# Fused attention and two MLPs: quarter tiles in the first stage, scores of all groups ahead, fourth group of the first tile turned sooner

## The chip, the cores and the metric

One core of a Trainium2 chip runs the whole program. The metric is the time of one execution on the device, in microseconds (us).

## The reference

Attention on q, k and v of shape 8 x 8 x 576 x 64 (batch, heads, tokens, head width), within chunks of 64 tokens, and then two MLPs on the 4608 x 512 result:

```
scores = (q_c @ k_c.T) / sqrt(64)          # per head and chunk: 64 x 64
attn   = exp(scores - max); attn /= sum(attn) + 1e-9
x      = attn @ v_c                        # heads side by side: 4608 x 512
x      = relu(x @ w_in)**2 @ w_out         # 512 -> 2048 -> 512
h      = x @ w2_in
g      = where(h >= 1, h, where(h <= -1, 0, (h + 1)**2 / 4))
out    = g @ w2_out
```

## The kernel before

**Tiles and groups.** The 4608 tokens are nine tiles (TILES) of 512. A tile has four groups (GROUPS) of 128 tokens, a group has two chunks. Every large product is made of three passes, since each operand is held as a high part (HI, rounded to fp32r) and a low part (LO, the rest): ScalarE writes the high part, VectorE (for weights GpSimd) subtracts it to get the low one. In an MLP the hidden width is 16 slices (FT) of 128. `up` (L392) makes one slice of the hidden layer in one of two PSUM banks (`h_ps`), ScalarE takes relu and square (L689, L693, L694), VectorE the low part (`hid_lo`, L917), and `down` (L430) adds the slice's part of the output into the four banks of `acc`. up of the next slice is issued ahead of down of the one before. Phase 0 is the first MLP (tiles 0 to 8), phase 1 the second.

**Attention inside the tiles.** While tile t goes through the first MLP, the attention of tile t + 1 is made in its gaps, a group in four slices: exponentials on ScalarE (L632), `normalise` on VectorE (L876), `turn_probs` (L888, eight 32-row transposes of the probabilities in two halves, part 0 and part 1), then `heads_and_scores` on TensorE: 16 matmuls of 64x64 for the head outputs (L507; each f32 matmul shows as two instructions) and 16 for the scores of the next group (L520). VectorE's `turn` (L813) transposes q and k of the next groups, 16 transposes cut up by TURNS. In tile 0 the steps are laid out by STEPS_OF_FIRST_TILE, and its fourth group has parts 0 and 1 in one slice, f = 13. There VectorE runs in this order: normalise; hid_lo of slice 13; turn_probs part 0; nine transposes of q and k; hid_lo of slice 14; turn_probs part 1; four transposes; hid_lo of slice 15. TensorE's heads wait for the second half of turn_probs, and the scores behind them for the transposes of q and k and for hid_lo of slice 15.

**The first stage.** Before there is an MLP to hide it, the attention of groups 0 to 3 (tile 0) and the scores of group 4 are made with TensorE as transposer. After the matmuls of `keep_up` and a warming loop (L443, L572) the program order of TensorE is written out by hand: `turn(g)` (L462) transposes q and k of a group into acc banks 0 and 1; `score(g)` (L473) makes the scores into one bank, `s_ps`, as 8 matmuls of 128 x 64 x 128: k is stored zero-padded, so that q of two heads meets the even head's k and the odd head's k side by side (`qk_t` with three planes: q, even k, odd k). ScalarE copies q (L641) and the odd heads' half of k (L645), VectorE the even half (`copy_k`, L822). VectorE takes the maximum (`take_max`, L834) and subtracts it (`shift`, L841), ScalarE exponentiates (L651), VectorE sums (L849) and inverts (L866, L868), GpSimd normalises groups 0 to 2 (L324) and VectorE group 3 (L876). TensorE turns the probabilities (`turn_probs`, L486), ScalarE copies the two 64-row halves onto the diagonal blocks of a zeroed tile (`copy_turned`, L661; the second half of group 3 is VectorE's, L967), and `head_out` (L534) multiplies with v, 8 matmuls of 128 x 64 x 128. The result goes into `x_t`: high part on ScalarE (L679), low part on VectorE (L780), which count up x_hi and x_lo.

The order of TensorE is: score(0), turn(1), score(1), turn(2), turn_probs(0), score(2), turn(3), turn_probs(1), head_out(0), score(3), head_out(1), turn_probs(2), turn(4), up_half(0, 0), turn_probs(3), head_out(2), head_out(3), up_half(1, 0), up_half(0, 1), score(4), up_half(1, 1). `up_half(f, part)` (L403) is half of up for slice f, on the tokens of groups 0 and 1 (part 0) or 2 and 3 (part 1), 12 matmuls. up_half(0, 0) waits for x_lo of groups 0 and 1 and for w_in slice 0; up_half(1, 0) for w_in slice 1. Then down of slice 0 begins, which waits for its hid_lo.

**Buffers.** Probabilities are in `probs` (even groups) and `probs_spare` (odd groups), the turned ones in the upper half of `v_and_probs` and in `raw`. q and k of group 2 arrive in two parts of `stage`, which is also where the weights land (w_in slices in planes 0 and 2, w_out in 1 and 3).

**Queues.** GpSimd issues the weight loads and does their low parts (L313, L318), in one written order with the normalisations; its first load waits for the second turning (`k_turned`). SP issues q, k and v. ScalarE casts the weights' high parts (L616, L622), in its own written order: weights_in(0) between the heads of groups 0 and 1, weights_in(1) right after copy_turned(2).

## Time and profile before

| | |
|---|---|
| Time, median of 3 runs | 1646.14 us (1645.05 to 1646.54) |
| The profiled execution | 1645.59 us, of which the span of the profile is 1643.8 us |
| TensorE busy | 1635.7 us, 9354 matmul instructions |
| VectorE, ScalarE, GpSimd busy | 870.5, 597.3, 130.5 us |
| Granted TensorE clock | 1.00 (full) in all slices of the span |

Times in the rows are microseconds from the span's start. A row of a timeline merges instructions of one kind that follow each other: start, length, engine, line, operation, output <- inputs, shapes and count; in square brackets the idle time of the engine before it and what ended it. PE is TensorE's matmuls and PEld its weight loads, DVE VectorE, ACT ScalarE, POOL GpSimd, SP SyncE. The busy share of an engine says little by itself here; what counts is which wait ends last at a given place.

### The profile page before, as it was taken

How to read it: one execution, taken by the hardware profiler on the slowest of the kernel's cores; microseconds unless marked ns; L12 is line 12 of the kernel's file. 1: busy time of each engine (PE TensorE's matmuls, PEld its weight loads, DVE VectorE, ACT ScalarE, POOL GpSimd, SP SyncE). 2: the span in 40 equal slices, each digit the busy share in tenths (PEclk: the TensorE clock that was granted, in tenths of full speed). 3: DMA queues.
4: the chain of work that ended last, by engine and by line, in shares of the span. 5: the costliest groups of instructions: out<-in, count | busy, mean ns of one | idle time of the engine just before them, and what ended most of it. 6: DMA issues, size and time to landing. Idle time of an engine off the chain costs nothing.

```text
span 1643.8 us, 24537 instructions
## 1 busy us (share of the span) xinstructions
PE 1635.7 (100%) x9354; PEld 1350.7 (82%) x9354; DVE 870.5 (53%) x1628; ACT 597.3 (36%) x1409; POOL 130.5 (8%) x138
## 2 busy tenths in 40 slices
PE   9999999999999999999999999999999999999999
PEld 8878888888888888888888888888888888888887
DVE  6777667666677666663124444443434344443433
ACT  5554444444444443444542222222222222222222
POOL 4740000000000000001660000000000000000000
PEclk9999999999999999999999999999999999999999
DMA  9532121112112121212321010101010101010000
GB/s 184 128 88 58 40 65 34 52 39 65 40 23 61 39 65 33 52 27 84 93 83 49 1 52 0 52 0 51 0 51 0 51 0 51 0 51 1 23 4 26
DMA packets 126654, 74.70 MB, mean 45 GB/s; under 512 B 115553, under 2 KB 115553, under 8 KB 124257
## 3 DMA queue, kind: packets, MB, share of 16 engines
q1 hardware_dynamic: 119328, 56.11, 12.9%
q0 software_dynamic: 5120, 16.78, 3.4%
q8 instruction: 63, 1.03, 0.3%
q10 hardware_dynamic: 2112, 0.52, 0.2%
q14 instruction: 31, 0.25, 0.1%
HBM read 54.53 MB, written 18.87 MB: 45 GB/s over the span
## 4 chain that ended last, share of the span: by engine, by line
PE 98%; DVE 1%; issue 0%; ACT 0%; POOL 0%; POOLq 0%; DVEq 0%
PE _out_and_h_and_scores_ps L392 47%; PE acc L434 24%; PE acc L430 24%; PE _out_and_h_and_scores_ps L507 1%; PE _out_and_h_and_scores_ps L520 1%; DVE q_t_and_k_t_by_head L813 0%; PE _out_and_h_and_scores_ps L403 0%; PE _out_and_h_and_scores_ps L473 0%; DVE v_and_probs_diag L888 0%; PE _out_and_h_and_scores_ps L443 0%; PE acc L486 0%; PE acc L462 0%; PE _out_and_h_and_scores_ps L572 0%; PE _out_and_h_and_scores_ps L534 0%; DVE hidden_split L917 0%
## 5 line engine op out<-in xcount | busy, mean ns | idle before, releaser
L392 PE MATMUL _out_and_h_and_scores_ps<-x_t_split,w_in_split 128*128 128x512 f32 x3432 | 819.3, 389 | 0.1
L392 PEld LDWEIGHTS _out_and_h_and_scores_ps<-x_t_split,w_in_split 128*128 128x128 f32 x3432 | 644.0, 188 | 134.6 <-DVE x_t_split L787 0.9
L430 PE MATMUL acc<-hidden_split,w_out_split 128*128 128x512 f32 x1728 | 419.6, 392 | 1.0 <-DVE hidden_split L917 1.0
L434 PE MATMUL acc<-w_out_split,hidden_split 128*128 128x512 f32 x1728 | 414.7, 389 | 0.0
L434 PEld LDWEIGHTS acc<-w_out_split,hidden_split 128*128 128x128 f32 x1728 | 324.3, 188 | 67.3
L430 PEld LDWEIGHTS acc<-hidden_split,w_out_split 128*128 128x128 f32 x1728 | 321.7, 188 | 69.5 <-issue 1.5
L909 DVE SCALAR_TENSOR_TENSOR hidden_raw<-hidden_raw 128x512 f32<-128x512 f32 x144 | 99.7, 692 | 348.9 <-ACT hidden_raw L698 348.9
L813 DVE STREAM_TRANSPOSE q_t_and_k_t_by_head<-qk_in 32x256 f32<-32x256 f32 x496 | 216.0, 435 | 7.4
L698 ACT ACTIVATE hidden_raw<-_out_and_h_and_scores_ps 128x512 f32<-128x512 f32 x144 | 86.1, 598 | 364.9 <-PE _out_and_h_and_scores_ps L392 364.9
L917 DVE TENSOR_TENSOR hidden_split<-_out_and_h_and_scores_ps,hidden_split 128x512 fp32r<-128x512 f32 x144 | 99.6, 692 | 219.9 <-ACT _out_and_h_and_scores_ps L694 219.3
L689 ACT ACTIVATE _out_and_h_and_scores_ps<-_out_and_h_and_scores_ps 128x512 f32<-128x512 f32 x144 | 83.8, 582 | 359.2 <-PE _out_and_h_and_scores_ps L392 357.2
L702 ACT CAST hidden_split<-hidden_raw 128x512 fp32r<-128x512 f32 x144 | 89.3, 620 | 214.3 <-DVE hidden_raw L912 212.2
L917 DVE TENSOR_TENSOR hidden_split<-hidden_raw,hidden_split 128x512 fp32r<-128x512 f32 x144 | 99.8, 693 | 99.5 <-ACT hidden_split L702 99.5
L888 DVE STREAM_TRANSPOSE v_and_probs_diag<-probs 32x256 f32<-32x256 f32 x256 | 111.4, 435 | 3.6
L912 DVE TENSOR_TENSOR hidden_raw<-_out_and_h_and_scores_ps,hidden_raw 128x512 f32<-128x512 f32 x144 | 99.5, 691 | 4.9
L693 ACT ACTIVATE hidden_split<-_out_and_h_and_scores_ps 128x512 fp32r<-128x512 f32 x144 | 86.4, 600 | 4.8
L694 ACT ACTIVATE _out_and_h_and_scores_ps<-_out_and_h_and_scores_ps 128x512 f32<-128x512 f32 x144 | 85.5, 594 | 0.0
L632 ACT ACTIVATE probs<-_out_and_h_and_scores_ps,exp_bias 128x64 f32<-128x64 f32 x248 | 74.1, 325 | 29.1 <-DVE exp_bias L860 29.1
L300 POOL DMA_DIRECT2D qk_in<-in_moe_w_in_dram x16 | 12.3, 768 | 632.4 <-DVE q_t_and_k_t_by_head L813 628.2
L632 ACT ACTIVATION_READ_ACCUMULATOR probs<-_out_and_h_and_scores_ps,exp_bias 128x1 f32 x248 | 53.9, 217 | 0.0
L855 DVE TENSOR_REDUCE score_max<-_out_and_h_and_scores_ps 128x8 f32<-128x512 f32 x31 | 21.4, 692 | 41.3 <-PE _out_and_h_and_scores_ps L520 41.3
L674 ACT CAST x_t_split<-_out_and_h_and_scores_ps 128x512 fp32r<-128x512 f32 x32 | 18.8, 586 | 51.6 <-PE _out_and_h_and_scores_ps L507 51.6
(80 smaller groups left out, 493.2 us busy)
## 6 DMA issues: line engine op xcount, KB each, us to landing
v_and_probs_diag<-in_v_dram SPq DMA_DIRECT2D x72, 128.0 KB, 3.0
mlp_out_t<-stage SPq DMA_DIRECT2D x9, 1024.0 KB, 4.3
v_and_probs_diag<-mlp_out_t SPq DMA_DIRECT2D x9, 1024.0 KB, 6.9
qk_in<-in_q_dram SPq DMA_DIRECT2D x68, 128.0 KB, 3.1
qk_in<-in_k_dram SPq DMA_DIRECT2D x68, 128.0 KB, 3.1
out_dram<-stage SPq DMA_DIRECT2D x8, 1024.0 KB, 5.2
stage<-in_moe_w_in_dram POOLq DMA_DIRECT2D x16, 256.0 KB, 3.3
stage<-in_moe_w_out_dram POOLq DMA_DIRECT2D x16, 256.0 KB, 3.0
```

The costliest lines, as they stand in the source:

```text
L392: last = nc.tensor.matmul(h_ps[:, bank, :], w_in[:, kt, w, cols], x_t[:, par, x, kt, :], start=(kt == 0 and w == HI and x == HI), stop=(kt ...
L430: last = nc.tensor.matmul(acc[:, j, :], w_out[:, f, w, cols], hid[:, half, x, :], start=first, stop=end)
L434: last = nc.tensor.matmul(acc[:, j, :], hid[:, half, w, cols], w_out[:, f, x, :], start=first, stop=end)
L632: last = nc.scalar.activation(probs_of(n)[:, pair, keys], scores[:, head % 2, pair, :], ACT.Exp, scale=SCALE, bias=bias[:, par, head:head ...
L693: nc.scalar.activation(hid[:, half, HI, :], squares, ACT.Square).then_inc(hid_hi, 1)
L698: nc.scalar.activation(raw[:, half, :], h_ps[:, half, :], ACT.Relu, bias=0.5, scale=0.5).then_inc(relu_done, 1)
L702: nc.scalar.copy(hid[:, half, HI, :], squares).then_inc(hid_hi, 1)
L813: last = nc.vector.transpose(dst, src)
L888: last = nc.vector.transpose(probs_diag[at:at + BLK, :, tok * BLK:(tok + 1) * BLK], heads[tok * BLK:(tok + 1) * BLK, :, wid * BLK:(wid + 1 ...
L909: nc.vector.scalar_tensor_tensor(out=a, in0=a, scalar=1.0, in1=a, op0=ALU.min, op1=ALU.mult).then_inc(squared, 1)
L912: nc.vector.tensor_tensor(a, h_ps[:, half, :], a, ALU.max).then_inc(raw_ready, 1)
L917: nc.vector.tensor_tensor(hid[:, half, LO, :], squares, hid[:, half, HI, :].bitcast(F32), ALU.subtract).then_inc(hid_lo, 1)
```

## The change

It rewrites the first stage, and moves one step in tile 0.

- k is stored unpadded (`qk_t` has two planes), the turned probabilities too. Scores and heads of the first stage use the 64 x 64 quarter tiles which the later tiles use already (`scores`, `heads`), 16 matmuls each, into pairs of banks. Nothing has to be zeroed.
- Each group 0 to 3 has a buffer of its own for its probabilities (`probs`, two of `probs_spare`, plane 3 of `stage`); q and k of group 2 arrive in `raw`.
- TensorE's order is now: score(0), turn(1), score(1), turn(2), score(2), turn(3), score(3), turn_probs(0), head_out(0), turn_probs(1), head_out(1), turn_probs(2), up_half(0, 0), turn_probs(3), head_out(2), turn(4), head_out(3), up_half(1, 0), up_half(0, 1), score(4), up_half(1, 1). Head outputs of groups 0 and 1 share one pair of banks, those of groups 2 and 3 another, and scores of groups 0 to 3 one.
- ScalarE copies q and all of k from group 1 on; VectorE copies k of group 0 alone. The written orders of ScalarE, VectorE and GpSimd follow; load_in(0) waits for the third turning, load_out(1) for turn_probs(2).
- In tile 0, shift(4) comes ahead of hid_lo of slice 0. Where parts 0 and 1 fall in one slice (the fourth group, f = 13), turn_probs part 0 comes right behind normalise, ahead of hid_lo.

The core of the diff; left out are the renaming of PSUM banks (same banks for the later tiles), of semaphores, and the moves of functions without a change in what they issue.

```diff
-        v_and_probs = sb("v_and_probs_diag", [P, 4, H * D])
+        v_and_probs = sb("v_and_probs_t", [P, 4, H * D])
...
-        probs_diag = v_and_probs[:, 2:4, :].rearrange("p a (h n) -> p (a h) n", n=P)
-        qk_t = sb("q_t_and_k_t_by_head", [P, HP, 3, P])
+        qk_t = sb("q_t_and_k_t", [P, HP, 2, P])
         probs = sb("probs", [P, HP, P])
-        probs_spare = sb("probs_spare", [P, HP, P])
+        probs_spare = sb("probs_spare", [P, 2, HP, P])
...
         def probs_of(n):
-            return probs_spare[:] if spare(n) else probs[:]
-
-        def probs_diag_of(n):
-            return raw[:].rearrange("p a (h n) -> p (a h) n", n=P) if spare(n) else probs_diag
+            if isinstance(n, int) and 1 <= n < GROUPS:
+                return stage[:, 3, :].rearrange("p (hp n) -> p hp n", n=P) if n == 2 else probs_spare[:, n // 2, :, :]
+            return probs[:]
+
+        def probs_t_of(n):
+            place = 3 if isinstance(n, int) and n < GROUPS and n % 2 == 1 else 2
+            return v_and_probs[:, place, :].rearrange("p (h n) -> p h n", n=CHUNK)
...
         def qk_of(g):
             if g == 2:
-                return stage[:, 1:4:2, :]
+                return raw[:]
             return qk_in[:, 0 if g in (0, 3) else 1, :, :]
...
+        def pair(first):
+            return banks[:, first:first + 2, 0:TILE // 2].rearrange("p a (hp n) -> p a hp n", n=CHUNK)
...
+        def early_scores(n):
+            return pair(2 if n == GROUPS else 6)
+
+        def early_heads_out(n):
+            return pair(4 if n < 2 else 3)
...
-            nc.gpsimd.memset(probs_diag_of(1), 0.0).then_inc(spare_zero, 1)
-            pool.wait_ge(k_turned, 2)
+            pool.wait_ge(k_turned, 3)
             load_in(0, 0, stage)
             normalise(0, 0)
+            load_in(1, 0, stage)
             normalise(1, 1)
-            load_in(1, 0, stage)
+            load_out(0, 0, stage)
             normalise(2, 0)
             weights_in(0, 0, stage)
-            pool.wait_ge(k_turned, 3)
-            load_out(0, 0, stage)
             load_in(2, 0, stage)
+            weights_in(1, 0, stage)
+            pool.wait_ge(p_turned, 3)
             load_out(1, 0, stage)
-            weights_in(1, 0, stage)
             load_in(3, 0, stage)
             weights_out(0, 0, stage)
             load_out(2, 0, stage)
...
+                if f == 1:
+                    pe.wait_ge(shifted, GROUPS)
...
+                    if not past(s, 1) and j == 2:
+                        pe.wait_ge(shifted, GROUPS + 1)
...
-                if g > 0:
-                    pe.wait_ge(q_copied, g)
-                    pe.wait_ge(k_copied, g)
-                for which, turned in ((0, q_turned), (1, k_turned)):
+                for which, turned, copied in ((0, q_turned, q_copied), (1, k_turned, k_copied)):
+                    if g > 0:
+                        pe.wait_ge(copied, g)
...
+            def scores(place):
+
+                for hp in range(HP):
+                    for r in range(2):
+                        head_rows = slice(r * D, (r + 1) * D)
+                        for c in range(2):
+                            rows = slice(c * CHUNK, (c + 1) * CHUNK)
+                            last = nc.tensor.matmul(place[rows, r, hp, :], qk_t[head_rows, hp, 0, rows],
+                                                    qk_t[head_rows, hp, 1, rows], start=True, stop=True)
+                last.then_inc(scored, 1)
...
+            def early_score(n):
                 pe.wait_ge(q_copied, n + 1)
                 pe.wait_ge(k_copied, n + 1)
+                if n == GROUPS:
+                    pe.wait_ge(p_copied, n)
+                    pe.wait_ge(x_lo, n)
+                elif n > 0:
+                    pe.wait_ge(shifted, n)
+                scores(early_scores(n))
...
+            def early_head_out(n):
+                pe.wait_ge(p_copied, n + 1)
                 if n > 0:
-                    pe.wait_ge(shifted, n)
-                for hp in range(HP):
-                    for c in range(2):
-                        rows = slice(c * CHUNK, (c + 1) * CHUNK)
-                        last = nc.tensor.matmul(s_ps[rows, hp, :], qk_t[:, hp, 0, rows], qk_t[:, hp, 1:3, rows],
-                                                start=True, stop=True)
-                last.then_inc(scored, 1)
+                    pe.wait_ge(x_lo, n)
+                heads(n, early_heads_out(n))
...
             keep_up(WARM[2])
-            for g in range(GROUPS):
-                score(g)
-                if g + 1 < GROUPS:
-                    turn(g + 1)
-                    if g == 0:
-                        keep_up(WARM[3])
-                    if g >= 1:
-                        turn_probs(g - 1)
-                    if g >= 2:
-                        head_out(g - 2, g % 2)
-            head_out(1, 1)
+            early_score(0)
+            turn(1)
+            keep_up(WARM[3])
+            early_score(1)
+            turn(2)
+            early_score(2)
+            turn(3)
+            early_score(3)
+            turn_probs(0)
+            early_head_out(0)
+            turn_probs(1)
+            early_head_out(1)
             turn_probs(2)
-            turn(GROUPS)
             up_half(0, 0)
             turn_probs(3)
-            head_out(2, 0)
-            head_out(3, 1)
+            early_head_out(2)
+            turn(GROUPS)
+            early_head_out(3)
             up_half(1, 0)
             up_half(0, 1)
-            score(GROUPS)
+            early_score(GROUPS)
...
-                nc.scalar.copy(qk_t[:, :, 0, :], acc[:, 0, :].rearrange("p (hp n) -> p hp n", hp=HP))
+                nc.scalar.copy(qk_t[:, :, 0, :], acc[:, 0, :].rearrange("p (hp n) -> p hp n", hp=HP)).then_inc(q_copied, 1)
+
+            def copy_k(g):
                 act.wait_ge(k_turned, g + 1)
-                if g == 0:
-                    act.wait_ge(k_zero, 1)
-                nc.scalar.copy(qk_t[D:2 * D, :, 2, :], acc[D:2 * D, 1, :].rearrange(
-                    "p (hp n) -> p hp n", hp=HP)).then_inc(q_copied, 1)
+                nc.scalar.copy(qk_t[:, :, 1, :], acc[:, 1, :].rearrange("p (hp n) -> p hp n", hp=HP)).then_inc(k_copied, 1)
...
-            def copy_turned(n, chunks=(0, 1)):
+            def copy_turned(n):
                 act.wait_ge(p_turned, n + 1)
                 if n >= 2:
                     act.wait_ge(headed, n - 1)
-                else:
-                    act.wait_ge(spare_zero if spare(n) else probs_diag_zero, 1)
-                for c in chunks:
-                    rows = slice(c * CHUNK, (c + 1) * CHUNK)
-                    last = nc.scalar.copy(probs_diag_of(n)[rows, :, rows], acc[rows, 2, :].rearrange("p (h n) -> p h n", n=CHUNK))
-                last.then_inc(p_copied, 1)
+                nc.scalar.copy(probs_t_of(n), acc[:, 2, :].rearrange("p (h n) -> p h n", n=CHUNK)).then_inc(p_copied, 1)
...
             copy_q(0)
-            for g in range(GROUPS):
-                if g + 1 < GROUPS:
-                    copy_q(g + 1)
-                if g == GROUPS - 1:
-                    x_in_hi(0, 0, 0)
-                    weights_in(0, 0, stage)
-                    x_in_hi(1, 0, 1)
-                exponentiate(g)
-                if g >= 1:
-                    copy_turned(g - 1)
+            copy_q(1)
+            copy_k(1)
+            exponentiate(0)
+            copy_q(2)
+            copy_k(2)
+            exponentiate(1)
+            copy_q(3)
+            copy_k(3)
+            exponentiate(2)
+            copy_turned(0)
+            heads_in_hi(0, 0, 0, early_heads_out(0))
+            exponentiate(3)
+            copy_turned(1)
+            weights_in(0, 0, stage)
+            heads_in_hi(1, 0, 1, early_heads_out(1))
+            copy_turned(2)
+            copy_turned(3)
+            heads_in_hi(2, 0, 2, early_heads_out(2))
             weights_in(1, 0, stage)
-            copy_turned(3, (0,))
-            x_in_hi(2, 0, 2)
-            x_in_hi(3, 0, 3)
+            heads_in_hi(3, 0, 3, early_heads_out(3))
+            copy_q(GROUPS)
+            copy_k(GROUPS)
...
             def shift(n):
                 dve.wait_ge(maxed, n + 1)
-                if n >= 2:
-                    dve.wait_ge(p_turned, n - 1)
-                nc.vector.tensor_tensor(probs_of(n).rearrange(by_head, n=CHUNK), s_ps.rearrange(by_head, n=CHUNK),
-                                        top[:].unsqueeze(2).to_broadcast([P, H, CHUNK]), ALU.subtract).then_inc(shifted, 1)
+                if n == GROUPS:
+                    dve.wait_ge(p_turned, 1)
+                nc.vector.tensor_tensor(
+                    probs_of(n).rearrange("p hp (r n) -> p r hp n", r=2), early_scores(n),
+                    top[:].rearrange("p (hp r) -> p r hp", r=2).unsqueeze(3).to_broadcast([P, 2, HP, CHUNK]),
+                    ALU.subtract).then_inc(shifted, 1)
...
                         normalise(n, g % 2)
+                        if 1 in parts:
+                            turn_probs(n, 0)
+                    if attends and begins:
+                        shift(n)
...
                     if attends and begins:
-                        shift(n)
                         turn(t, 1, 1, TURNS[0], TURNS[1])
...
                     for r in (1, 2):
-                        if attends and r in parts:
+                        if attends and r in parts and 0 not in parts:
                             turn_probs(n, r - 1)
...
-            nc.vector.memset(qk_t[:, :, 1:3, :], 0.0).then_inc(k_zero, 1)
-            nc.vector.memset(probs_diag, 0.0).then_inc(probs_diag_zero, 1)
-            dve.wait_ge(k_zero, 1)
-
-            copy_k(0)
+            dve.wait_ge(k_turned, 1)
+            nc.vector.tensor_copy(qk_t[:, :, 1, :], acc[:, 1, :].rearrange("p (hp n) -> p hp n", hp=HP)).then_inc(k_copied, 1)
             for g in range(GROUPS):
                 take_max(g)
                 shift(g)
-                if g + 1 < GROUPS:
-                    copy_k(g + 1)
-                    add_up(g, g % 2)
-                    invert(g, g % 2)
-            x_in_lo(0, 0, 0)
-            x_in_lo(1, 0, 1)
+                if g >= 1:
+                    add_up(g - 1, (g - 1) % 2)
+                    invert(g - 1, (g - 1) % 2)
+            heads_in_lo(0, 0, 0, early_heads_out(0))
             add_up(3, 1)
             normalise(3, 1)
-            dve.wait_ge(p_turned, 4)
-            dve.wait_ge(headed, 2)
-            nc.vector.tensor_copy(probs_diag_of(3)[CHUNK:P, :, CHUNK:P],
-                                  acc[CHUNK:P, 2, :].rearrange("p (h n) -> p h n", n=CHUNK)).then_inc(last_p_copied, 1)
-            copy_k(GROUPS)
-            x_in_lo(2, 0, 2)
-            x_in_lo(3, 0, 3)
-            copy_q_of_fifth()
+            heads_in_lo(1, 0, 1, early_heads_out(1))
+            heads_in_lo(2, 0, 2, early_heads_out(2))
+            heads_in_lo(3, 0, 3, early_heads_out(3))
```

## Rows read from the trace of the kernel before

**Rows 1.** Busy time of each engine in three stretches (length, busy, instructions; PEclk, DMA share, GB/s)

```profile
core 0: us, PE busy (x) PEld busy (x) DVE busy (x) ACT busy (x) POOL busy (x), PEclk, DMA share, GB/s
200.00:800.00 600.00, 600.00 (x4073) 493.09 (x4072) 390.23 (x843) 260.78 (x747) 18.81 (x21) 1.00 0.19 49
11.50:23.95 12.45, 11.28 (x205) 10.09 (x204) 10.47 (x22) 10.04 (x18) 6.85 (x8) 1.00 0.90 176
109.70:124.30 14.60, 12.90 (x115) 10.15 (x114) 13.27 (x31) 6.64 (x22) 3.71 (x3) 1.00 0.08 19
```

**Rows 2.** Timeline of TensorE in the first stage (start, length)

```profile
1.54 2.50 PE L443 MATMUL _out_and_h_and_scores_ps<-ident 128*128 128x128 f32 x10 [1.54 <-POOL ident L329]
...
8.95 1.09 PE L473 MATMUL _out_and_h_and_scores_ps<-q_t_and_k_t_by_head 128*64 128x128 f32 x16 [0.27 <-DVE q_t_and_k_t_by_head L822]
9.97 1.10 PE L462 MATMUL acc<-ident,qk_in 128*128 128x128 f32 x8
...
19.94 1.04 PE L473 MATMUL _out_and_h_and_scores_ps<-q_t_and_k_t_by_head 128*64 128x128 f32 x16
...
23.70 1.69 PE L403 MATMUL _out_and_h_and_scores_ps<-x_t_split,w_in_split 128*128 128x256 f32 x12
25.47 1.15 PE L486 MATMUL acc<-ident,probs_spare 128*64 128x64 f32 x32
...
28.48 3.17 PE L403 MATMUL _out_and_h_and_scores_ps<-x_t_split,w_in_split 128*128 128x256 f32 x24
...
34.33 3.00 PE L430 MATMUL acc<-hidden_split,w_out_split 128*128 128x512 f32 x12
```

**Rows 3.** Timeline of VectorE and TensorE around the fourth group of tile 0

```profile
105.79 0.69 DVE L876 TENSOR_TENSOR probs<-probs,prob_sum_inverse 128x512 f32<-128x512 f32 x1
...
109.07 0.69 DVE L917 TENSOR_TENSOR hidden_split<-_out_and_h_and_scores_ps,hidden_split 128x512 fp32r<-128x512 f32 x1 [2.59 <-ACT _out_and_h_and_scores_ps L694]
...
111.46 4.03 DVE L813 STREAM_TRANSPOSE q_t_and_k_t_by_head<-qk_in 32x256 f32<-32x256 f32 x9
...
115.50 0.69 DVE L917 TENSOR_TENSOR hidden_split<-_out_and_h_and_scores_ps,hidden_split 128x512 fp32r<-128x512 f32 x1
...
116.34 3.00 PE L430 MATMUL acc<-hidden_split,w_out_split 128*128 128x512 f32 x12 [0.95 <-DVE hidden_split L917]
...
119.88 0.69 DVE L917 TENSOR_TENSOR hidden_split<-_out_and_h_and_scores_ps,hidden_split 128x512 fp32r<-128x512 f32 x1
...
120.72 0.69 PE L520 MATMUL _out_and_h_and_scores_ps<-q_t_and_k_t_by_head 64*64 64x64 f32 x32 [0.75 <-DVE hidden_split L917]
```

**Rows 4.** Timeline of TensorE: quarter tiles inside tile 0

```profile
53.58 0.69 PE L507 MATMUL _out_and_h_and_scores_ps<-v_and_probs_diag 64*64 64x64 f32 x32
54.10 0.65 PE L520 MATMUL _out_and_h_and_scores_ps<-q_t_and_k_t_by_head 64*64 64x64 f32 x32
```

**Rows 5.** Timeline of ScalarE in the first stage

```profile
10.67 0.59 ACT L641 COPY q_t_and_k_t_by_head<-acc 128x512 f32<-128x512 f32 x1 [2.05 <-PE acc L462]
...
21.90 0.59 ACT L679 CAST x_t_split<-acc 128x512 fp32r<-128x512 f32 x1 [0.25 <-PE acc L534]
...
22.48 0.63 ACT L651 ACTIVATE probs_spare<-probs_spare 128x512 f32<-128x512 f32 x1
...
24.20 0.62 ACT L616 CAST w_in_split<-stage 128x512 fp32r<-128x512 f32 x1
...
31.69 0.58 ACT L689 ACTIVATE _out_and_h_and_scores_ps<-_out_and_h_and_scores_ps 128x512 f32<-128x512 f32 x1 [1.99 <-PE _out_and_h_and_scores_ps L403]
```

**Rows 6.** Timeline of VectorE in the first stage

```profile
10.81 0.69 DVE L841 TENSOR_TENSOR probs<-_out_and_h_and_scores_ps,score_max 128x512 f32<-128x512 f32 x1
...
22.96 0.68 DVE L780 TENSOR_TENSOR x_t_split<-acc,x_t_split 128x512 fp32r<-128x512 f32 x1
...
33.49 0.69 DVE L917 TENSOR_TENSOR hidden_split<-_out_and_h_and_scores_ps,hidden_split 128x512 fp32r<-128x512 f32 x1
```

**Rows 7.** Timeline of GpSimd: low part of one w_in slice

```profile
21.73 1.28 POOL L313 TENSOR_TENSOR w_in_split<-stage,w_in_split 128x512 fp32r<-128x512 f32 x1
```

**Rows 8.** Instructions of L300 (w_in loads) in the first 45 us: their landing times

```profile
DMA to landing us min/median/max: 3.2/4.5/6.3
```

124 lines of the change are left out of this document (38 added, 86 removed).

## The prediction, made before the change was run

> **What bounds the kernel now.** I read the stretches first, to see where TensorE has room. In the long middle it has none: it is busy 600.00 of 600.00 us, at the granted clock 1.00, which is the 2.4 GHz level [rows 1]. So nothing the change does on other engines can be seen there, and any microsecond lost or won before or between the dense blocks goes through to the end whole. The change touches two places. The first is the opening stage (attention of groups 0 to 3), which ends when the first down projection starts at 34.33 us [rows 2]; from 11.50 to 23.95 us TensorE is busy 11.28 of 12.45 us [rows 1], so the room there is about 1.2 us of idling plus whatever work is removed. The second is the fourth group in tile 0, where TensorE stands twice, 0.95 and 0.75 us, each time released by VectorE's hid_lo at L917 [rows 3]; the stretch around it is busy 12.90 of 14.60 us [rows 1]. Then I read the timeline of each engine for durations.
>
> **First stage, front half: the scores run ahead.** A padded score takes 1.09 us, and the turning behind it starts 1.02 later (8.95 and 9.97) [rows 2]. Quarter tiles, the form that L507 and L520 already have, take 0.69 and 0.65 us, the next starts 0.52 and 0.57 us after them [rows 4]. I take 0.57 for a score or a head_out. The opening up to score(0) at 8.95 is the same: the copy of k still sits on VectorE there, and the zeroing that is removed (DVE, POOL) was done before its operands arrived. Then, per group: the turning starts 0.57 after the score; ScalarE's copy of q starts 0.70 after the turning (9.97, 10.67) [rows 2, 5]; it now copies q and the whole of k one behind the other, 0.59 + 0.02 each (before, VectorE took half of k in parallel, but ScalarE's half cost it as much); 0.1 to TensorE. That is 0.57 + 0.70 + 1.20 + 0.10 = 2.57 per group. Scores of groups 1, 2, 3 start at 11.5, 14.05, 16.6 us; before, the last of them stood at 19.94 [rows 2]. VectorE's subtraction takes 0.69 [rows 6], and I give the max the same; they are done 2.1 us after a score starts, so they don't gate this cycle.
>
> **First stage, middle.** turn_probs(0) now stands behind score(3): 17.15 to 18.30 (1.15, as [rows 2] have it). From there TensorE has nothing to do in its written order but follow ScalarE's: copy_turned(0) to 18.93; head_out(0) 19.1 to 19.8; heads_in_hi(0), 0.59 [rows 5], to 20.4; then exponentiate(3), 0.63 [rows 5], which was ready at 18.7 but is queued behind it, to 21.04; copy_turned(1) to 21.65; head_out(1) 21.8 to 22.5; heads_in_hi(1) to 23.12; heads_in_lo(1), 0.68 [rows 6], to 23.85; up_half(0, 0) at 23.95. Before it started at 23.70 [rows 2]. So 3.3 us of lead in the scores are given back, and 0.25 us more. The cast of w_in(0), which waits for its transfer, is not in this way: load_in(0) is moved behind the third turning (to 13.2 us), its slowest landing is 6.3 us [rows 8], so it is there at about 19.6 to 20.5, and ScalarE asks for it at 21.67. Should the landing be later than that, each microsecond of it goes onto the end. SP's queue keeps its order; v and the fifth group are issued when they were, or earlier.
>
> **First stage, tail.** Before, TensorE was nearly dense from 25.47 to 34.33 us. Now: up_half(0, 0) to 25.5 (24 of these matmuls take 3.17, the last 0.07 beside what follows, so 12 take 1.55) [rows 2]; turn_probs(3) to 26.65; head_out(2); turn(4), which is moved to here and costs 1.1 (the eight matmuls at 9.97), to 28.3. head_out(3) has to wait, since groups 2 and 3 now share one place in PSUM: copy_turned(3) 26.7 to 27.3, heads_in_hi(2) to 27.97, heads_in_lo(2) to 28.7, so it starts at 28.8: **0.5 us idle**. ScalarE casts w_in(1) only behind heads_in_hi(2): 28.0 to 28.61 (0.62) [rows 5], GpSimd's part takes 1.28 [rows 7], so up_half(1, 0) starts at 30.0 instead of 29.4: **0.6 us idle**; it started at 28.48 before [rows 2]. Then up_half(0, 1) 31.6 to 33.15, and the relu at L689 follows at 33.2 (31.69 before) [rows 5]. Its hid_lo would be ready at 35.0, by the 1.80 us between 31.69 and 33.49 [rows 5, 6], but shift(4) is moved ahead of it on VectorE: score(4) at 33.15, max 33.88 to 34.57, subtraction to 35.28, hid_lo 35.3 to 36.0, down(0, 0) at 36.1. The first stage ends **1.8 us later** than at 34.33. The new wait at j = 2 of down(0, 0) and the one ahead of up_half(1) are long met. Moved later on POOL: load_out(1), to about 30.3, because weights_in(1) stands in front of it; with a landing of up to 6.3 us [rows 8] it is there at 36.6 to 37, just where ScalarE wants it (about 36.1), and down(0, 1) wants it at 41.8: I cost it at nothing, covered by 3 us.
>
> Bounds of this part: if the two idle spots of the tail and the shift are hidden after all, and the middle breaks even, +0.3; if each of some fourteen handovers costs 0.1 us more than I gave it, +3.2. I take 1.8, since all of its terms are durations of the same operations in this trace.
>
> **Fourth group of tile 0.** Before, VectorE ended its normalisation at 106.48 (105.79 + 0.69) and idled until hid_lo(13), then did four transposes of probabilities and nine of q and k at 0.45 each, and reached hid_lo(14) at 115.50, hid_lo(15) at 119.88 [rows 3]. The change puts the first four into that idle time: 106.5 to 108.3, while hid_lo(13) cannot start before 109.07, when the squares are ready. So all that follows moves up by 1.75: hid_lo(14) is over at 114.5, before TensorE asks for it at about 115.3 (116.34 less the wait), and the wait of 0.95 and its refill (1.0 to 1.1 in all) are gone; hid_lo(15) ends at 118.9, and the score starts at 119.0 instead of 120.72, with 0.4 us of standing left, the next late one. **Gain 1.7 us**. Above, it is bounded by the two waits with their refills, 2.0; below by 1.0, if only the first wait goes.
>
> **Sum.** 1.8 - 1.7 = +0.1 us on the profiled execution's 1645.59 (span 1643.8). The median of the runs is 1646.14, 0.55 above it, so I forecast 1646.2. About 0.2% (3.3 us) is what a measurement of this kernel can tell from no change; I expect this one not to show.
>
> **The rivals.**
> (a) *The lead is kept.* The fourth group's score comes 3.3 us sooner, TensorE's work after 25.47 shrinks a little, and the fourth group gives 1.7: 3.3 + 0.2 + 1.7 = 5.2 us, 1640.9. For it speaks that before the scores and the VectorE steps behind them stood in the chain; against it the written order of ScalarE, where exponentiate(3) stands behind heads_in_hi(0), and the casts of w_in(1). Chance 0.07.
> (b) *The stage breaks even*, since handovers are shorter than I gave or idle spots overlap: only the 1.7 us are left, 1644.4. Chance 0.17.
> (c) *Slower, by TensorE's clock.* In the stretch from 11.50 to 23.95 TensorE falls from 11.28 us busy to 8.5 (2 turnings at 1.1, 3 scores and 2 heads at 0.57, 3 turn_probs at 1.15), with pauses up to 1 us. The opening shows the price: ten matmuls of 128x128 take 2.50 us, 250 ns each, against 1.10 / 8 = 138 ns at 9.97 [rows 2], although the records give 1.00 for the whole run. If it fell back to the 1.2 GHz level at about 14 us, the TensorE pieces on the path to 23.95 (0.57 + 0.70 + 0.57 + 1.15 + 0.65 + 0.65, about 4.3 us) take twice that, and if up_half(0, 0) and turn_probs(3) are still slow, their 2.7 us cost as much again: +7, 1653. It decides from the point where TensorE, with these pauses, is taken to the lower level; against it, no pause by my sum is above 1.1 us. Chance 0.07. The Trainium skill ("TensorE: Matmul & The Clock Gate", Part 1: The HAM clock gate) says that the half rate is the default and activity releases it; by that rule this stage would get nearer to the half rate, and the sum would be the 1653 of this rival. The trace of before shows no fall back, so I don't follow it.
> (d) *The change does little of what it says*: quarter tiles run no faster here, and the fourth group's wait moves elsewhere. The stage then ends 2 us later than I said, no gain: 1650. Chance 0.04.
>
> **How the numbers follow.** My case has 0.65; its own range is +0.3 - 2.0 to +3.2 - 1.0, so 1644.4 to 1648.3 around the median. With the scatter of the runs shown (-1.1, +0.4) and case (b) this gives 1643.2 to 1649.2, leaving out (a), (c) and (d). Faster by over 0.2% is (a) with the edge of (b): 0.08; slower (c), (d) and the edge of mine: 0.11; the rest, 0.81, is the same.
>
> **What would show it.** Right: scores of group 3 at about 16.6 us; TensorE idle 0.8 us before each of head_out(0) and head_out(1); up_half(0, 0) at 24; idle before head_out(3) and, released by POOL, before up_half(1, 0); down(0, 0) at 36; one wait of about 0.4 us left at the fourth group's score, none at its down projection. Wrong: down(0, 0) at or before 34.3, DMA named as releaser on ScalarE or TensorE, matmuls of 128x128 at 250 ns behind 14 us, or a new wait on weights in tile 0.

## The result and the profile after

| | before | this |
|---|---|---|
| median (lowest to highest), 14 runs each | 1645.73 us (1644.96 to 1646.74) | 1649.01 us (1646.92 to 1650.51) |
| ratio, 95% interval | | 1.0019 (1.0011 to 1.0027) |
| profiled execution, its span | 1645.59, 1643.8 | 1648.3, 1646.5 |
| down(0, 0) starts, first stage over | 34.33 | 38.55 |
| score of the fourth group in tile 0 | 120.72 | 123.23 |

The changed kernel is about 3.3 us slower, which is 0.2%. The interval lies above 1, so the loss does show, though the prediction expected a change too small to be told. Forecast was 1646.2: the measured time is inside the range of 1643.2 to 1649.2, near its upper end, and 2.8 us above the forecast. In the profiles the first stage grew by 4.2 us where 1.8 was worked out; the fourth group gave back 1.7 us, as worked out.

TensorE's timeline of the first stage, from the scores of group 3, beside [rows 2]:

```profile
16.49 0.69 PE L487 MATMUL banks<-q_t_and_k_t 64*64 64x64 f32 x32 [0.77 <-ACT q_t_and_k_t L641]
17.12 1.15 PE L516 MATMUL banks<-ident,probs 128*64 128x64 f32 x32
18.96 0.69 PE L476 MATMUL banks<-v_and_probs_t 64*64 64x64 f32 x32 [0.68 <-ACT v_and_probs_t L652]
19.58 1.15 PE L516 MATMUL banks<-ident,probs_spare 128*64 128x64 f32 x31
22.50 0.22 PE L516 MATMUL banks<-ident,probs_spare 128*64 128x64 f32 x1 [1.77 <-issue]
23.39 0.74 PE L476 MATMUL banks<-v_and_probs_t 64*64 64x64 f32 x32 [0.68 <-ACT v_and_probs_t L652]
24.06 1.97 PE L516 MATMUL banks<-ident,stage 128*64 128x64 f32 x32
25.96 2.29 PE L403 MATMUL banks<-x_t_split,w_in_split 128*128 128x256 f32 x12
28.19 1.15 PE L516 MATMUL banks<-ident,probs_spare 128*64 128x64 f32 x32
...
31.44 0.69 PE L476 MATMUL banks<-v_and_probs_t 64*64 64x64 f32 x32 [0.46 <-issue]
32.58 3.11 PE L403 MATMUL banks<-x_t_split,w_in_split 128*128 128x256 f32 x24 [0.45 <-issue]
...
38.55 2.98 PE L432 MATMUL banks<-hidden_split,w_out_split 128*128 128x512 f32 x12 [0.60 <-DVE hidden_split L897]
```

Read the fifth line first. turn_probs(1) is 32 recorded matmuls with no wait among them, yet TensorE does 31, stands for 1.77 us and does the last. The releaser is "issue": nothing that the profile shows held the engine. (The name alone proves little: the 0.46 and 0.45 us further down have it too, and there the last operand is ready a tenth of a microsecond before TensorE goes on, at 31.34 us from VectorE and at 32.48 us from GpSimd. What counts here is that the program has no wait between these 32 matmuls.) Then turn_probs(2) takes 1.97 us where turn_probs(3), two lines below it, takes 1.15 for 32 matmuls of the same shape, and up_half(0, 0) takes 2.29 us. The windows say what they have in common (length, then busy time and count of PE, PEld, DVE, ACT and POOL, then the granted clock, the DMA share and GB/s), beside [rows 1]:

```profile
11.50:23.95 12.45, 7.54 (x239) 6.32 (x228) 9.39 (x20) 6.18 (x12) 5.31 (x7) 1.00 1.04 189
24.16:27.57 3.41, 3.41 (x40) 3.29 (x41) 0.69 (x1) 1.17 (x2) 1.83 (x2) 0.54 0.44 108
113.88:128.48 14.60, 14.29 (x122) 11.59 (x121) 13.23 (x31) 8.19 (x27) 3.73 (x3) 1.00 0.09 20
```

In the second, TensorE never idles and its granted clock is 0.54, which is close to the 1.2 GHz level; the kernel before shows no such stretch. The third holds the fourth group, which comes 4.18 us later here, so the window is moved by as much: busy 14.29 of 14.60 us, where it was 12.90. Its rows, VectorE's first, beside [rows 3]:

```profile
109.99 0.69 DVE L852 TENSOR_TENSOR probs<-probs,prob_sum_inverse 128x512 f32<-128x512 f32 x1
110.72 1.77 DVE L864 STREAM_TRANSPOSE v_and_probs_t<-probs 32x256 f32<-32x256 f32 x4
113.25 0.69 DVE L897 TENSOR_TENSOR hidden_split<-banks,hidden_split 128x512 fp32r<-128x512 f32 x1 [0.76 <-ACT banks L680]
113.97 4.03 DVE L800 STREAM_TRANSPOSE q_t_and_k_t<-qk_in 32x256 f32<-32x256 f32 x9
...
119.41 2.88 PE L432 MATMUL banks<-hidden_split,w_out_split 128*128 128x512 f32 x12
...
123.23 0.69 PE L487 MATMUL banks<-q_t_and_k_t 64*64 64x64 f32 x32 [0.31 <-DVE hidden_split L897]
```

The four transposes stand in what was idle time and still leave 0.76 us of it; the down projection has no wait any more, and 0.31 us is left at the score.

TensorE stands from 20.73 to 22.50 us. What moves shortly before that is seen in the DMA view of the 0.2 us slice from 19.6 us, at the start of turn_probs(1):

```profile
DMA packets 177, 0.06 MB, mean 316 GB/s; under 512 B 175, under 2 KB 175, under 8 KB 176
q1 hardware_dynamic: 171, 0.04, 108.2%
q8 instruction: 1, 0.02, 40.9%
```

One packet of the instruction queue, 0.02 MB, begins here, and TensorE goes on 2.7 to 2.9 us later. In the kernel before the like packet begins at 19.2 to 19.4 us, but TensorE has its 345th matmul record only at about 25.8 us. Here that record is the one before the stop, and ends at 20.73.

### The profile page after: what moved, and what is told of

Read it like the earlier page. It is cut to its first block, busy times and chain, and to the rows that moved or that the text cites. A ratio compares the mean times of both kernels' runs of the same rounds, so it can differ in the third digit from the quotient of the medians.

```text
span 1646.5 us, 24807 instructions
## 1 busy us (share of the span) xinstructions
PE 1634.5 (99%) x9498; PEld 1349.6 (82%) x9498; DVE 864.8 (53%) x1619; ACT 595.5 (36%) x1407; POOL 129.3 (8%) x137
## 4 chain that ended last, share of the span: by engine, by line
PE 98%; DVE 1%; issue 0%; DMA 0%; ACT 0%; SPq 0%; POOL 0%; POOLq 0%; DVEq 0%
PE banks L390 47%; PE banks L436 24%; PE banks L432 24%; PE banks L476 1%; PE banks L487 1%; PE banks L516 0%; PE banks L403 0%; DVE q_t_and_k_t L800 0%; DMA qk_in<-in_k_dram 0%; PE banks L464 0%; PE banks L446 0%; DVE hidden_split L897 0%; SPq L206 0%; PE banks L567 0%; DVE v_and_probs_t L864 0%
## 5 line engine op out<-in xcount | busy, mean ns | idle before, releaser
L390 PE MATMUL banks<-x_t_split,w_in_split 128*128 128x512 f32 x3432 | 819.4, 389 | 0.1
L390 PEld LDWEIGHTS banks<-x_t_split,w_in_split 128*128 128x128 f32 x3432 | 643.9, 188 | 134.7 <-DVE x_t_split L775 0.9
L432 PE MATMUL banks<-hidden_split,w_out_split 128*128 128x512 f32 x1728 | 419.5, 392 | 0.6 <-DVE hidden_split L897 0.6
L436 PE MATMUL banks<-w_out_split,hidden_split 128*128 128x512 f32 x1728 | 414.7, 389 | 0.0
L436 PEld LDWEIGHTS banks<-w_out_split,hidden_split 128*128 128x128 f32 x1728 | 324.4, 188 | 67.4
L432 PEld LDWEIGHTS banks<-hidden_split,w_out_split 128*128 128x128 f32 x1728 | 321.8, 188 | 68.8 <-issue 0.8
L800 DVE STREAM_TRANSPOSE q_t_and_k_t<-qk_in 32x256 f32<-32x256 f32 x496 | 215.9, 435 | 7.4
L897 DVE TENSOR_TENSOR hidden_split<-banks,hidden_split 128x512 fp32r<-128x512 f32 x144 | 99.6, 692 | 218.1 <-ACT banks L680 217.6
L675 ACT ACTIVATE banks<-banks 128x512 f32<-128x512 f32 x144 | 83.8, 582 | 359.8 <-PE banks L390 358.3
L864 DVE STREAM_TRANSPOSE v_and_probs_t<-probs 32x256 f32<-32x256 f32 x256 | 111.3, 435 | 3.6
L680 ACT ACTIVATE banks<-banks 128x512 f32<-128x512 f32 x144 | 85.5, 594 | 0.0
L831 DVE TENSOR_REDUCE score_max<-banks 128x8 f32<-128x512 f32 x31 | 21.4, 692 | 41.3 <-PE banks L487 41.3
```

The source lines that it names most:

```text
L390: last = nc.tensor.matmul(h_ps[:, bank, :], w_in[:, kt, w, cols], x_t[:, par, x, kt, :], start=(kt == 0 and w == HI and x == HI), stop=(kt ...
L432: last = nc.tensor.matmul(acc[:, j, :], w_out[:, f, w, cols], hid[:, half, x, :], start=first, stop=end)
L436: last = nc.tensor.matmul(acc[:, j, :], hid[:, half, w, cols], w_out[:, f, x, :], start=first, stop=end)
L800: last = nc.vector.transpose(dst, src)
L864: last = nc.vector.transpose(probs_t_of(GROUPS)[at:at + BLK, :, tok % 2 * BLK:(tok % 2 + 1) * BLK], heads[tok * BLK:(tok + 1) * BLK, :, wi ...
L897: nc.vector.tensor_tensor(hid[:, half, LO, :], squares, hid[:, half, HI, :].bitcast(F32), ALU.subtract).then_inc(hid_lo, 1)
```

## The experiments

Two theories went in. **Supply:** TensorE ran out of instructions, since the change lets it reach the end of a block of its program sooner, while a crowd of transfers holds the next block back. **Clock:** the pauses of rival (c) pull it to the half rate, and fewer pauses would keep it up.

### The two edits apart

The kernel before with the fourth group's edit alone:

```diff
                         normalise(n, g % 2)
+                        if 1 in parts:
+                            turn_probs(n, 0)
...
-                        if attends and r in parts:
+                        if attends and r in parts and 0 not in parts:
                             turn_probs(n, r - 1)
```

> The kernel before with the one step moved in tile 0 (first half of turn_probs ahead of hid_lo of slice 13), and nothing else. My sum: TensorE's wait of 0.95 us before the down projection of slice 14 is gone, the one before the fourth group's score falls from 0.75 to about 0.3, median 1.7 us under before (ratio 0.9990). Rival, the move only shifts the wait to the weights or to ScalarE: ratio 1.000.

Measured: 1643.76 us (1643.34 to 1644.36, 11 runs), ratio 0.9989 (0.9980 to 0.9998): 1.97 us less. VectorE and TensorE in the profile:

```profile
106.50 1.78 DVE L888 STREAM_TRANSPOSE v_and_probs_diag<-probs 32x256 f32<-32x256 f32 x4
115.24 2.88 PE L430 MATMUL acc<-hidden_split,w_out_split 128*128 128x512 f32 x12
119.07 0.69 PE L520 MATMUL _out_and_h_and_scores_ps<-q_t_and_k_t_by_head 64*64 64x64 f32 x32 [0.32 <-DVE hidden_split L919]
```

The wait of 0.95 us is gone, the one of 0.75 is 0.32. This is the term of 1.7 us, seen by itself, at the upper end of what it was given (2.0).

The changed kernel with that edit undone (the same lines the other way round):

> The changed kernel without the moved step in tile 0. If the two parts add up: 1.7 us above the changed kernel, so 5.0 us above before (ratio 1.0030), with the first down projection at 38 to 39 us and both waits of before in the fourth group. If they interact through the transfers or the weights: a difference to the changed kernel under 1 us or over 2.5 us.

Measured: 1650.42 us (1648.11 to 1651.78, 8 runs), ratio 1.0026 (1.0016 to 1.0037): 4.69 us more than before, and 1.41 more than the changed kernel, so the two edits roughly add up. In its profile the stop stands at the same matmul, for 3.41 us, the instruction packet begins at 21.2 to 21.4 instead of 19.6 to 19.8 us, and down(0, 0) starts at 39.93, later than the 38 to 39 expected. So the first stage alone carries the loss, and the length of the stop differs between executions, since up to there the two kernels issue the same.

### Is it the crowd of transfers?

The first down projection's weights are issued later on GpSimd:

```diff
             normalise(1, 1)
-            load_out(0, 0, stage)
             normalise(2, 0)
             weights_in(0, 0, stage)
+            load_out(0, 0, stage)
```

> The changed kernel with the first w_out load issued behind the low part of w_in slice 0 (about 25 us) instead of at 18.0 us, so that fewer transfers run while TensorE turns the probabilities of group 1. Theory 1, the idle time of 1.8 us inside that run of matmuls is a late load of TensorE's own instructions, held up behind data transfers: it shrinks below 0.5 us, the first down projection comes at about 36.5 us, and the median falls 1.5 to 2.5 us under the changed kernel's. Theory 2, TensorE has simply used up its instructions there, whatever the data transfers do: idle time 1.5 us or more at the same matmul, median unchanged within 0.5 us.

Measured: 1648.47 us (1646.85 to 1650.27, 11 runs), ratio 1.0016 (1.0007 to 1.0025). The stop is there, 2.04 us, and the median is 0.54 us under the changed kernel's, within the scatter of both. This one 256 KB load isn't what matters.

The fifth group's q and k, which come in small packets (175 of 177 in the slice above are under 512 bytes), are issued later by SP:

```diff
             sp.wait_ge(k_turned, 2)
-            load_early_qk(4, qk_loaded[1])
             load_v(2, 0)
+            load_early_qk(4, qk_loaded[1])
             load_v(3, 1)
```

> The changed kernel with the four transfers of q and k of the fifth group issued behind the first transfer of v of group 2 (about 21 us) instead of from 13.4 us on; they are asked for at about 29 us. It takes away half a megabyte of data transfers that stand in the engines' queues while TensorE's second load of instructions is due. Theory 1 (the load is held up behind data): the load starts at 17 to 18.5 us instead of 20.0, the idle time inside turn_probs of group 1 is under 0.5 us, no half clock behind it, the first down projection at 36 to 36.5 us, median 2 to 3 us under the changed kernel's. Theory 2 (the load is asked for late, whatever the data do): load at 20 to 21 us, idle time 1.5 us or more, median within 0.5 us of the changed kernel's.

Measured: 1646.59 us (1645.97 to 1651.0, 10 runs), ratio 1.0007 (0.9998 to 1.0016). Nine of the ten lie within 1645.97 to 1647.22, the tenth, at 1651.0, is the only one with a mean granted clock under 1. In the profile the instruction packet begins at 18.0 to 18.2, in a slice with six packets, and the stop is short:

```profile
19.12 1.15 PE L516 MATMUL banks<-ident,probs_spare 128*64 128x64 f32 x31
20.75 0.22 PE L516 MATMUL banks<-ident,probs_spare 128*64 128x64 f32 x1 [0.48 <-issue]
...
22.27 1.15 PE L516 MATMUL banks<-ident,stage 128*64 128x64 f32 x32
23.77 1.70 PE L403 MATMUL banks<-x_t_split,w_in_split 128*128 128x256 f32 x12 [0.35 <-DVE x_t_split L775]
...
35.98 2.98 PE L432 MATMUL banks<-hidden_split,w_out_split 128*128 128x512 f32 x12 [0.60 <-DVE hidden_split L897]
```

```profile
DMA packets 6, 0.03 MB, mean 143 GB/s; under 512 B 2, under 2 KB 2, under 8 KB 5
q8 instruction: 1, 0.02, 36.1%
```

turn_probs(2) is back at 1.15 us. With the stop nearly gone, up_half(0, 0) starts at 23.77 and down(0, 0) at 35.98, where the prediction had 23.95 and 36.1. Part of that agreement is the opening, which ends sooner in this execution: over the eleven profiles of this case score(0) starts anywhere from 7.82 to 9.00 us, here at 8.15. Counted from score(0), down(0, 0) comes 27.83 us later, against 25.38 before, 29.81 in the changed kernel and 27.15 in the prediction's sum. So the sum is 0.68 us short here, and 0.48 of that is the stop. In medians this kernel is 0.78 us above the 1645.81 of before measured beside it. The profile is of the fastest of its ten runs.

### Is it the number of instructions?

The 32 small matmuls of the warming loop (64 records) become four large ones (8 records), so that fewer instructions stand ahead of the stage:

```diff
             keep_up(WARM[0])
-            for i in range(2 * HP):
-                for r in range(2):
-                    for c in range(2):
...
+            keep_up(4)
```

> The changed kernel with the 64 small matmuls of the warming loop replaced by 8 large ones that take the same 2.0 us, so 56 matmuls fewer stand before the place at which TensorE runs out of instructions (so far always behind matmul 345). If it is a place in the program: the idle time moves 56 matmuls later, into turn_probs of group 2 at 22 us, where the load has landed or nearly; idle time under 0.5 us, median 1.5 to 3 us under the changed kernel's. If it is a moment in time (about 20.7 to 22.5 us), or belongs to turn_probs of group 1: it stays where it is, same median.

Measured: 1645.64 us (1645.24 to 1649.12, 10 runs), ratio 1.0001 (0.9992 to 1.0011), 3.37 us under the changed kernel, more than the 1.5 to 3 expected. Nothing stops in turn_probs(1). A short stop appears in turn_probs(0), behind matmul record 218:

```profile
16.90 0.92 PE L516 MATMUL banks<-ident,probs 128*64 128x64 f32 x24
18.22 0.45 PE L516 MATMUL banks<-ident,probs 128*64 128x64 f32 x8 [0.40 <-issue]
...
19.97 1.15 PE L516 MATMUL banks<-ident,probs_spare 128*64 128x64 f32 x32
21.81 0.69 PE L476 MATMUL banks<-v_and_probs_t 64*64 64x64 f32 x32 [0.69 <-ACT v_and_probs_t L647]
22.43 1.16 PE L516 MATMUL banks<-ident,stage 128*64 128x64 f32 x32
...
36.80 2.98 PE L432 MATMUL banks<-hidden_split,w_out_split 128*128 128x512 f32 x12 [0.60 <-DVE hidden_split L892]
```

In this profile up_half(0, 0) waits 1.24 us for another reason: VectorE's normalise(3) at 22.49 us takes 1.69 us instead of 0.69, beside GpSimd's low part of w_in (22.35 to 23.62), and holds up the low part of x behind it.

The places where TensorE stops, 218 and 345 (the latter in the changed kernel and the three runs above), are 127 records apart, and each matmul has a weight load beside it: some 254 instructions. The Trainium skill ("Advanced Engine Details and Errata", ISA Cache) gives blocks of 16 KB, 256 instructions; spacing and packet size here agree with it. In the changed kernel record 218 is the last of turn(3), where TensorE waits 0.77 us for ScalarE anyway, which would hide a stop there. The end of the block at 345 now lies in turn_probs(2), at about 23.1 us, 3.0 us after the packet of 20.0 to 20.2. No transfer was moved here, so this run is the better evidence for supply.

### Is it the pauses?

Nine matmuls on `ident` into the free bank 3 (the expectation says 11) fill TensorE's idle places:

```diff
             turn(2)
+            keep_up(2, 3)
             early_score(2)
             turn(3)
+            keep_up(2, 3)
             early_score(3)
             turn_probs(0)
+            keep_up(2, 3)
             early_head_out(0)
             turn_probs(1)
+            keep_up(3, 3)
             early_head_out(1)
```

> The changed kernel with 2 or 3 matmuls on the identity (into a free bank) put into each of the four idle places of TensorE between 13 and 22 us, 11 more in all. Clock theory: the stretch at half clock from 23.9 to 27.3 us is gone in the profile (128x256 matmuls of the first half slice in 1.7 instead of 2.3 us), median 0.8 to 1.2 us under the changed kernel's. Instruction theory adds: the idle place of 1.8 us moves to an earlier step or changes its length, since 44 more instructions of TensorE come before it. If neither holds: same median, same idle place, same half clock.

Measured: 1657.06 us (1655.65 to 1658.84, 5 runs), ratio 1.0066 (1.0053 to 1.0080). The fillers didn't keep the clock: it fell during the stop, which is longer here.

```profile
18.71 0.80 PE L516 MATMUL banks<-ident,probs_spare 128*64 128x64 f32 x19
23.60 0.91 PE L516 MATMUL banks<-ident,probs_spare 128*64 128x64 f32 x13 [4.09 <-issue]
24.44 1.65 PE L446 MATMUL banks<-ident 128*128 128x128 f32 x6
...
27.09 1.97 PE L516 MATMUL banks<-ident,stage 128*64 128x64 f32 x32
```

The stop moved from behind the 31st matmul of turn_probs(1) to behind the 19th, by the twelve records of the fillers that now stand ahead of it: it hangs on the count of instructions and not on this operation. The packet begins at 20.8 us here, 1.3 us after TensorE had stopped; why so late isn't in the trace.

In medians this kernel is 8.05 us above the changed one. Its profile is of the slowest of its five runs, 10.5 us above the changed kernel's, and only 2.5 of these are in the first stage (down(0, 0) at 41.08). The rest hadn't been expected. It is in the second MLP, where TensorE stops twice in the middle of its dense stream, for 2.76 us behind record 7200 and for 3.20 us behind record 7968, the latter followed by half clock. The second, with the window around it and the DMA view of the 0.2 us slice from 1298.0 us:

```profile
1294.89 2.88 PE L436 MATMUL banks<-w_out_split,hidden_split 128*128 128x512 f32 x12
1300.97 4.26 PE L390 MATMUL banks<-x_t_split,w_in_split 128*128 128x512 f32 x12 [3.20 <-issue]
```

```profile
1298.00:1306.00 8.00, 5.03 (x15) 4.02 (x16) 0.54 (x2) 0.60 (x1) 0.00 (x0) 0.79 0.02 4
```

```profile
DMA packets 1, 0.02 MB, mean 82 GB/s; under 512 B 0, under 2 KB 0, under 8 KB 0
q8 instruction: 1, 0.02, 38.1%
```

It is the same delay of supply: an instruction packet begins as TensorE stands (in the slices from 1120.6 and 1298.0 us), and TensorE goes on 2.6 to 3.0 us later. The packet is alone in its slice, and the DMA share of the window is 0.02, so no crowd of transfers makes this wait. The two places are 768 records apart, which is one pass of TensorE's loop over two tiles of the second MLP (2 tiles, 16 slices, 12 + 12 matmuls), and 7200 and 7968 are the ends of its first and second pass, where it jumps back. From 1100 to 1450 us the kernel before and the one with the short warming load no instruction packet at all; the changed kernel and this one load 18. So in the kernel before the loop goes round on what is loaded already, and in the changed one it doesn't. That this hangs on how many instructions stand ahead of the loop is seen from the short warming, which leaves the loop itself as it is. In the changed kernel the packets cost nothing that the profile shows (no stop at either jump), here two stops. What decides between these two isn't shown.

### A version that keeps the lead?

The short warming and the late q and k together, with the orders of TensorE, ScalarE and VectorE woven anew: turn_probs(1) into a bank of its own and ahead of head_out(0), and group 4 turned and scored behind up_half. The core of it on TensorE:

```diff
             turn_probs(0)
-            early_head_out(0)
             turn_probs(1)
+            early_head_out(0)
             early_head_out(1)
...
             early_head_out(2)
-            turn(GROUPS)
             early_head_out(3)
...
             up_half(0, 1)
-            early_score(GROUPS)
+            turn(GROUPS)
             up_half(1, 1)
+            early_score(GROUPS)
```

> A version that should beat both: the changed kernel with both edits above, and the written orders rearranged: turn_probs of group 1 into a bank of its own right behind that of group 0; a place of its own for each head output that needs one; ScalarE casts w_in of slice 1 ahead of copy_turned(3) and exponentiates group 3 behind the two casts of x; turning, copies, score, maximum and subtraction of the fifth group all behind the second half of up(0). By my sum, up_half(0, 0) at 22.5 us, no waits between up_half(1, 0) and down(0, 0), which starts at 33.1 us (before 34.33), and the 1.7 us of the fourth group: ratio 0.998 of before, 1642.8. If instruction loads still hold it up: down(0, 0) at 35 us or later, ratio 0.9993 or above.

Measured: 1651.90 us (1650.53 to 1652.5, 6 runs), ratio 1.0034 (1.0022 to 1.0046). One row tells it:

```profile
32.96 1.14 PE L476 MATMUL banks<-v_and_probs_t 64*64 64x64 f32 x32 [6.14 <-DMA v_and_probs_t<-in_v_dram]
```

v of group 3 stood behind q and k of group 4 in SP's queue, and half-clock matmuls followed; down(0, 0) starts at 42.08, where the sum had 33.1. Two more orders of that queue, all else the same: q and k of group 4 first, as in the change, and then behind v of groups 2 and 3.

> The rearranged version (e7) with q and k of the fifth group issued where the changed kernel has them, from 13.4 us on, so that v of group 3 no longer queues behind them. If the wait of 6.1 us for v of group 3 was that queue: it is gone, down(0, 0) at 33.7 to 34.5 us, median 1643.2 to 1644.2. If the second or third load of instructions is held up instead (as in the changed kernel, where these transfers ran at the same time): one or two idle places of over 1 us at matmuls 217 and 345, half clock behind them, median over 1645.

> The rearranged version (e7) with the transfers of q and k of the fifth group issued last, behind both of v of groups 2 and 3 (from about 23.5 us). No wait for v of group 3, instruction loads as short as in e7 (idle places of 0.7 and 0.9 us at most), turning of the fifth group at 30 us waits 1 us at most for its q and k; down(0, 0) at 33.5 to 34.5 us, median 1643.0 to 1644.2, the least of all if e8 is held up.

Measured: 1644.61 us (1643.33 to 1647.19, 11 runs), ratio 0.9994 (0.9985 to 1.0003), and 1645.00 us (1644.43 to 1647.57, 11 runs), ratio 0.9997 (0.9988 to 1.0006). Both profiles are of the slowest run of their kernel, 2.6 us above the median, so what they show is the bad case and not the usual one. The first has stops of 0.66 and of 2.54 us behind the same two records, the longer one here:

```profile
24.74 0.50 PE L516 MATMUL banks<-ident,stage 128*64 128x64 f32 x9 [2.54 <-issue]
```

The second has none. up_half(0, 0) starts at 21.93, 1.8 us sooner than before the change (0.9 of it from the opening, score(0) at 8.06 instead of 8.95), and two other waits take that back:

```profile
21.93 1.69 PE L403 MATMUL banks<-x_t_split,w_in_split 128*128 128x256 f32 x12 [0.28 <-DVE x_t_split L771]
24.77 1.15 PE L516 MATMUL banks<-ident,probs_spare 128*64 128x64 f32 x32 [1.16 <-DVE probs_spare L848]
...
29.00 1.07 PE L476 MATMUL banks<-v_and_probs_t 64*64 64x64 f32 x32 [2.45 <-DMA v_and_probs_t<-in_v_dram]
```

The wait of 6.14 us is gone in the first, so it was that queue; in the second 2.45 us of waiting for v of group 3 remain, though nothing of group 4 stands ahead of it, and its cause is open. The wait for probs_spare is the longer normalise(3) again, 1.70 us beside GpSimd's low part of w_in. down(0, 0) starts at 37.38 and 37.72 in these two, where 33.5 to 34.5 was hoped for, and the second, expected to be the fastest of all, is not. Neither is told apart from the kernel before. Of all that ran, the fourth group's edit alone is the fastest, and the only one whose interval lies below 1.

## Why the prediction was right, and where it was short

**First stage, front half: right.** Scores of group 3 at 16.49 us (16.6), turn_probs(0) at 17.12 (17.15), head_out(0) at 18.96 (19.1). The quarter tiles run as [rows 4] have them, 0.69 us for 32 records, so rival (d) is out.

**First stage, middle: this step failed.** It let TensorE follow ScalarE's written order and nothing else, and put the supply of TensorE's instructions at nothing. turn_probs(1) was to end at about 20.9 us with copy_turned(1) over at 21.65; it ended at 22.72, by the stop of 1.77 us, and up_half(0, 0) started at 25.96 instead of 23.95. The stop is 1.77 of it. The half clock adds 0.82 in turn_probs(2) (1.97 less 1.15), of which about 0.47 count (an estimate: at full clock up_half(0, 0) would have waited some 0.35 us for x_lo, as it did in the run with q and k later), and 0.59 in up_half(0, 0) (2.29 less 1.70). The missing term is 1.77 + 0.47 + 0.59 = 2.8 us. About 0.4 came back elsewhere: score(0) began 0.21 us sooner than in the profile of before, and the tail was 0.13 us shorter than worked out. That leaves the 2.45 between 38.55 and 36.1. With the stop nearly gone (q and k later) the step's own reading held: counted from score(0) the sum was 0.68 us short, 0.48 of it the stop.

**First stage, tail: right.** 0.46 us idle before head_out(3), 0.45 before up_half(1, 0), 0.60 before down(0, 0) with VectorE's low part as releaser, the three places that the sum had at 0.5, 0.6 and the shift. The first two bear the name "issue", but VectorE's low part of x ends at 31.34 and GpSimd's low part of w_in at 32.48, each a tenth of a microsecond ahead, as the sum had it. From up_half(1, 0) to down(0, 0) it is 5.97 us, worked out as 6.1.

**Fourth group: right.** From down(0, 0) to the score it was 86.39 us (120.72 less 34.33) and is 84.68: 1.71 gained against 1.7, 0.31 of waiting left against 0.4. Alone on the kernel before, 1.97 us.

**Rival (a)**, the lead is kept: no. ScalarE had exponentiate(3) at 20.20, behind the heads' high part at 19.72, in the order that spoke against it; with that order rewoven, other waits came. **Rival (b)**: no, the stage didn't break even. **Rival (c)**, slower by the clock: its slow matmuls are there, its mechanism is not. Before the stop, pauses of 0.77 and 0.68 us left the clock at 1.00 (the first window above); half clock came only behind the stop, for 3.41 us, and cost 0.47 + 0.59 = 1.1 us, not 7. Filling the pauses added to the instructions, and the kernel became slower. The rule weighed there (the Trainium skill, "TensorE: Matmul & The Clock Gate", Part 1: The HAM clock gate) would have had this stage nearer to the half rate as a whole; the trace has it so behind the long stop alone.

**The whole.** +4.2 in the first stage and -1.7 in the fourth group make +2.5, and the profiled executions differ by 2.7 (1648.3 less 1645.59). The medians differ by 3.3, since the profiled execution of the changed kernel is 0.7 us under its median. That the time fell inside the range is in part luck: the first stage alone, +4.2, is outside its own bounds of +0.3 to +3.2, and they were drawn for longer handovers and not for a stop. By the prediction's own figures the upper end is 1648.3 + 0.4 = 1648.7; it wrote 1649.2 without saying where the other 0.5 come from, and the 1649.01 lies between the two.

The profile of before had no stop, since it reached that matmul 5 us later. Its waits couldn't show that there was a margin to lose; the count of TensorE's instructions against the start of the instruction packet (record 345 at 25.8 us, packet at 19.2) could have.

## What to carry to other kernels

When an edit lets an engine run ahead, count its instructions as well as its work: many tiny matmuls in an opening stage can get to the end of the loaded instructions before the next block is there. In a profile this is idle time released by "issue" inside a run of one operation that waits for nothing, at the same count of instructions in each variant, with a packet of the instruction queue that began 2 to 3 us before TensorE goes on; in a loop, look at the jump back. Cut instructions rather than fill the pauses. Moving transfers of small packets away was followed by a shorter stop here too, but why isn't shown. Look also at where the profiled execution lies among the runs of its kernel: three of the profiles here are of the slowest run. And when two edits come together, time each alone: here the small one was worth 2 us, and the large one hid it.

## What the runs showed that was not expected

- TensorE's instructions can be late in straight-line code. The stops there were 0.40 to 4.09 us long, and TensorE went on 2.2 to 2.9 us after the instruction packet had begun, in the seven profiles with a stop behind record 345. The Trainium skill ("Runtime: NRT & Kernel Launch", Instruction fetch mechanics) has the next block fetched while the current one runs, and the cost of the boundary "mostly hidden"; here it was hidden in the kernel before and not in the changed one, where the 1.77 us are in the open.
- When the packet begins varies: 18.0 to 22.2 us over ten profiles. What asks for it isn't in the trace. That other transfers hold it back is supported by the run with q and k later (a tight group of times 2.4 us below the changed kernel's), but not proved: two woven kernels (q and k late, and last) with nearly the same first 20 us had it at 20.7 and at 18.0, and the two stops in the loop came with the DMA engines nearly idle. That the margin hangs on the count of instructions is shown twice, by the short warming and by the fillers.
- Half clock stood in the first stage behind stops or waits of 1.77 us and more (for 3.41 us in the changed kernel), and behind none of up to 1.24 us. In the loop it followed the stop of 3.20 us, and the one of 2.76 us left the clock at 1.00, so the length of a stop doesn't decide alone.
- Nine more matmuls in the opening brought two stops of about 3 us into a steady loop, at 1121 and 1298 us, at its two jumps back. The kernel before loads no instructions while it goes round there (none from 1100 to 1450 us), the changed kernel and all that have its opening load 18 packets, and those with the short warming none.
- VectorE's normalise(3) took 1.69 and 1.70 us instead of 0.69 in two profiles, where it started 0.1 us behind a GpSimd operation of 1.27 us (its low part of w_in). In the kernel before, where GpSimd started 0.2 us behind VectorE, GpSimd's took 1.64 us instead of 1.28. Where an edit moved the two onto each other, it cost a microsecond; the prediction had no term for it, and the changed kernel happens to avoid it.
